# Blockwise attention and a swish feed-forward on one core: batch 0 in two passes by queries, K back on SyncE

## The reference

```python
scores = scale * np.matmul(q, k.transpose(0, 1, 3, 2))
mask = block_i >= block_j                    # blocks of 64 positions
attn = softmax(np.where(mask, scores, -1e9))
x = np.matmul(attn, v).transpose(0, 2, 1, 3).reshape(4608, 512)
h = x @ w_in                                 # 512 x 2048
g = h * (1.0 / (1.0 + np.exp(-beta * h)))
out = g @ w_out                              # 2048 x 512
```

## Time and profile before

| | |
|---|---|
| median of 3 runs | 364.31 us (364.09 to 367.67) |
| the profiled execution | 364.09 us |
| its span | 362.3 us |
| mean granted clock of TensorE | 0.967 |
| TensorE busy | 332.3 us |
| VectorE, ScalarE, GpSimd busy | 218.2, 211.0, 82.4 us |
| DMA | 53.41 MB |

### The profile page before, as it was taken

The page is one execution under the profiler, slowest core; times in us unless marked ns, Lnnn a source line. Parts: engine busy times, 40 slices in busy tenths (PEclk is TensorE's granted clock), DMA queues, the critical chain, the costliest instruction groups (busy, mean ns, idle before and its releaser), DMA issues.

```text
span 362.3 us, 7406 instructions
## 1 busy us (share of the span) xinstructions
PE 332.3 (92%) x3104; PEld 205.7 (57%) x3048; DVE 218.2 (60%) x447; ACT 211.0 (58%) x320; POOL 82.4 (23%) x127
## 2 busy tenths in 40 slices
PE   7879959876998999999956999999999999999996
PEld 5465345432556644765533566656666676676685
DVE  4657735354574548855952567467648757757742
ACT  2938906126955669668552876775687636535521
POOL 6684066303601804203703333000000000000000
PEclk9999969996999999999995999999999999999999
DMA  8999999999999599999799786150231021020023
GB/s 211 205 250 225 227 217 212 202 200 251 182 210 238 99 226 235 210 205 235 162 201 213 145 187 101 50 121 18 78 50 49 18 78 57 2 87 31 0 90 116
DMA packets 113313, 53.41 MB, mean 147 GB/s; under 512 B 83568, under 2 KB 112768, under 8 KB 113280
## 3 DMA queue, kind: packets, MB, share of 16 engines
q1 hardware_dynamic: 91424, 32.06, 46.3%
q10 hardware_dynamic: 16288, 16.52, 17.0%
q0 software_dynamic: 5568, 4.36, 7.6%
HBM read 36.71 MB, written 9.44 MB: 127 GB/s over the span
## 4 chain that ended last, share of the span: by engine, by line
PE 69%; DVE 6%; SPq 6%; DMA 6%; ACT 4%; POOL 3%; ACTq 3%; issue 2%; POOLq 0%
PE PS L960 28%; PE PS L890 24%; PE PS L747 7%; SPq L534 5%; PE PS L695 5%; PE PS L996 4%; DVE gT L974 3%; ACTq L1017 2%; DMA OV<-in_v_dram 2%; DMA xT<-xq 2%; ACT E L709 2%; DMA Vs<-in_v_dram 1%; DVE xq L766 1%; DVE OV L857 1%; ACT th L970 1%
## 5 line engine op out<-in xcount | busy, mean ns | idle before, releaser
L960 PE MATMUL PS<-xT,w_in 128*128 128x512 bf16 x576 | 143.3, 388 | 5.2 <-ACT ost L1011 4.7
L970 ACT ACTIVATE th<-PS,beta 128x512 f32<-128x512 f32 x144 | 97.2, 696 | 69.0 <-PE PS L960 66.1
L974 DVE SCALAR_TENSOR_TENSOR gT<-th,PS 128x512 f16<-128x512 f32 x144 | 95.9, 681 | 54.2 <-ACT th L970 53.9
L709 ACT ACTIVATE E<-PS 128x1024 bf16<-128x1024 f32 x93 | 92.1, 1031 | 42.4 <-PE PS L695 39.2
L960 PEld LDWEIGHTS PS<-xT,w_in 128*128 128x128 bf16 x576 | 53.6, 99 | 61.9 <-issue 6.0
L890 PE MATMUL PS<-w_out,gT 128*128 128x256 f16 x512 | 63.9, 273 | 0.0
L890 PEld LDWEIGHTS PS<-w_out,gT 128*128 128x128 f16 x512 | 48.6, 98 | 12.7 <-issue 0.8
L656 POOL CAST QKn<-ST 128x640 bf16<-128x640 f32 x48 | 35.5, 740 | 81.7 <-DMA ST<-in_k_dram 67.7
L747 PE MATMUL PS<-Vn,E 128*128 128x65 bf16 x930 | 35.2, 198 | 12.2 <-DMA xT<-xq 6.8
L747 PEld LDWEIGHTS PS<-Vn,E 128*128 128x128 bf16 x930 | 33.5, 101 | 17.8 <-DMA xT<-xq 7.1
L695 PE MATMUL PS<-QKT 64*128 64x512 bf16 (+4 forms) x328 | 37.6, 300 | 2.3 <-ACT E L709 2.0
(11 more groups left out here) (61 smaller groups left out, 176.3 us busy)
## 6 DMA issues: line engine op xcount, KB each, us to landing
out_dram<-ost ACTq DMA_DIRECT2D x36, 256.0 KB, 2.4
Vs<-in_v_dram SPq DMA_DIRECT2D x24, 256.0 KB, 6.1
ST<-in_q_dram SPq DMA_DIRECT2D x8, 288.0 KB, 6.3
ST<-in_k_dram SPq DMA_DIRECT2D x8, 288.0 KB, 6.8
w_in<-in_moe_w_in_dram POOLq DMA_DIRECT2D x4, 512.0 KB, 10.1
w_out<-in_moe_w_out_dram POOLq DMA_DIRECT2D x4, 512.0 KB, 10.3
OV<-in_v_dram SPq DMA_DIRECT2D x4, 256.0 KB, 12.3
Vs<-in_v_dram SPq DMA_DIRECT2D x6, 128.0 KB, 8.0
```

What stands on the lines that cost most here:

```text
L709: return g.activation(E3[es_(te)][:, g0, :, :], PS[:, ps.slot:ps.slot + 2, :], ACT.Exp, scale=0.125)
L960: z = g.matmul(PS[:, ph.slot, :], w_in[:, c, 128 * j:128 * j + 128], xT[:, c, row % RX:row % RX + RC], start=(c == 0), stop=(c == 3))
L970: return g.activation(th[tt.slot][:], PS[:, ph.slot, :], ACT.Tanh, scale=beta[:, j:j + 1])
L974: return g.scalar_tensor_tensor(out=gT[tg.slot][:, j, :], in0=th[tt.slot][:], scalar=1.0, in1=PS[:, ph.slot, :], op0=ALU.add, op1=ALU.mult)
```

## The change

- V of batch 0 comes on SP alone, in whole key tiles of all heads: part 0 is tiles 0 and 1, part 1 is the others. GpSimd casts each part for each pair.
- QK products of batch 0 are cut into nine blocks of 128 to 320 columns, laid out so that the first group holds all that queries 0 to 255 need. Its tiles of zeros move with them (CLEAR).
- PV, reciprocal, product, transpose and copy of batch 0 are done for query tiles 0 and 1 first (which wait for the first exponential and part 0 of V alone), then for tiles 2 to 4.
- Chunk 0's inner products are done for rows 0 to 255 (half 0, from the first passes), then for rows 256 to 511, two slices j in one PSUM bank, with two tanh of 256 columns each.
- K of batches 2 to 7 goes out on SP, behind Q. Q and K may use either of the two buffers.
- Pieces 1, 2 and 3 of w_in wait for K of pair 2, K of pair 3 and part 0 of V of batch 0; w_out waits for the last K of batch 1 and has a priority ahead of the casts of the last pairs.
- Both copies of xT that ScalarE did for batch 0 go to VectorE.

```diff
--- before.py
+++ after.py
-        PARTS = [((0, 4, "SP", range(6)), (4, 8, "SP", range(2)), (4, 8, "POOL", range(2, 6)))] + [((0, 8, "SP", range(6)),)] * 7
+        PARTS = [(range(0, 2), range(2, 6))] + [(range(6),)] * 7
...
+        BLOCKS = [{0: [(0, 0, 256, 0), (1, 128, 256, 256), (2, 384, 512, 384)], 1: [(0, 256, 576, 0), (3, 384, 576, 320)],
+                   2: [(1, 256, 576, 0), (2, 256, 384, 320), (2, 512, 576, 448)], 3: [(4, 512, 576, 0)]},
+                  {0: [(0, 0, 512, 0)], 1: [(0, 512, 576, 448), (1, 128, 576, 0)],
+                   2: [(2, 256, 576, 0), (3, 384, 576, 320)], 3: [(4, 512, 576, 0)]}]
+        CLEAR = [[(0, 256), (320,), (320,)], [(0,), (0,), (0, 320)]]
...
-            wout.append(P.op("POOL", 1000, fwo, xfer=3150, dma=(f"d_wout{a}", 1), prio=-18 if a < 1 else 4.6))
...
-            for h0, h1, e, tt in PARTS[b]:
+            for part, tt in enumerate(PARTS[b]):
...
-                    def fv(g, e, ts=ts, t=t, b=b, h0=h0, h1=h1, i=i):
-                        d = Vn[t.slot] if e == "POOL" else Vs[ts.slot]
...
-                            return [g.dma_start(d[:, i, h0:h1, 0:64],
-                                                v[b, h0:h1, 128 * i:128 * i + 128, :].rearrange("h p d -> p h d"))]
+                            return [g.dma_start(d[:, i, :, 0:64],
...
-                        o = P.op("SP", 300 + 550 * n, fv, tiles=[ts], xfer=(1400 if b == 0 else 1200) * n,
-                                 prio=3.5 + 0.1 * (h0 > 0) if b == 0 else 4 * b + (3.5 if b < 2 else 0.5),
-                                 dma=["d_V", h0, 1])
-                        o.pkt = 90.0
-                    else:
-                        o = P.op("POOL", 150 + 1450 * n, fv, tiles=[t], xfer=1400 * n, prio=-30 if b == 0 else 4 * b + (3.5 if b < 2 else 0.5), dma=["d_VP", h0, 1])
...
+                    o = P.op("SP", 300 + 550 * n, fv, tiles=[ts], xfer=(1400 if b == 0 else 1200) * n,
+                             prio=3.5 if b == 0 else 4 * b + (3.5 if b < 2 else 0.5), dma=["d_V", part, 1])
...
-                n = 5 if 4 in tt else len(tt)
-                for g0 in range(h0, h1, 2):
...
-                        return g.tensor_copy(Vn[t.slot][:, 0:n, g0:g1, 0:64], Vs[ts.slot][:, 0:n, g0:g1, :])
...
+                for g0 in range(0, 8, 2):
...
+                        return g.tensor_copy(Vn[t.slot][:, t0:t1, g0:g0 + 2, 0:64], Vs[ts.slot][:, t0:t1, g0:g0 + 2, :])
+
+                    o = P.op("POOL", 60 + 120 * (t1 - t0), fw, deps=[*vs, *ones, *vzero], tiles=[ts, t],
+                             prio=4 * b + 0.5 - (38.5 - 5 * part) * (b < 1))
...
                         ts = whole[w] = P.tile("S8")
-                        ts.only = (w,)
 
...
-                        o = P.op("ACT" if w else "SP", QKI, fl, deps=[o for t in early6 for o in t.users] if b == QB else [],
+                        o = P.op("SP", QKI, fl, deps=[o for t in early6 for o in t.users] if b == QB else [],
                                  tiles=[ts], xfer=QKX, prio=u, dma=["d_S8", 0, 1])
...
-                        if w:
-                            o.after = ld["Q", u]
...
-                        blocks = {0: [(0, 0, 512, 0)], 1: [(0, 512, 576, 448), (1, 128, 576, 0)],
-                                  2: [(2, 256, 576, 0), (3, 384, 576, 320)], 3: [(4, 512, 576, 0)]}[g0]
-                        for t, q0, q1, off in blocks:
+                        for t, q0, q1, off in BLOCKS[b > 0][g0]:
...
                 o = P.op("PE", n, fq, deps=cps, tiles=pst + [tqk] + [te] * (b > 0),
-                         lat=n + 200, mode="row", prio=pr(u) + .1 + .1*(grp[0] >= 2))
+                         lat=n + 200, mode="row", prio=pr(u) + (.1 + .1*(grp[0] >= 2) if b else -9 * (grp[0] == 0)))
...
-                    x = P.op("ACT", act_t(1024), fe, deps=[o], tiles=[ps, te], lat=act_t(1024) + 93, prio=0)
...
+                    x = P.op("ACT", act_t(1024), fe, deps=[o], tiles=[ps, te], lat=act_t(1024) + 93,
+                             prio=-1 if b == 0 and g0 == 0 else 0)
...
+                    cl = CLEAR[b > 0][g0]
+
+                    def fz(g, e, g0=g0, te=te, cl=cl):
+                        a = E3[es_(te)][64:128, g0, :, cl[0]:cl[0] + 64]
+                        if len(cl) == 1:
+                            return g.memset(a, 0.0)
+                        return g.memset(bass.AP(a.tensor, a.offset, [a.ap[0], [512, 2], [cl[1] - cl[0], 2], [1, 64]]), 0.0)
+                    zs.append(P.op("DVE", 110 + 55 * len(cl), fz, deps=[x], tiles=[te], prio=-20))
...
-            def eblk(te, t, i, h):
-                if t == 4:
+            def eblk(te, t, i, h, b=b):
+                if b == 0 and t < 4:
+                    g0, off = {(0, 0): (0, 0), (0, 1): (0, 128), (0, 2): (1, 0), (0, 3): (1, 128), (0, 4): (1, 256),
+                               (1, 1): (0, 256), (1, 2): (2, 0), (1, 3): (2, 128), (1, 4): (2, 256), (2, 2): (2, 320),
+                               (2, 3): (0, 384), (2, 4): (2, 448), (3, 3): (1, 320), (3, 4): (1, 448)}[t, i]
+                    a = 1024 * g0 + 512 * h + off
+                elif t == 4:
...
-            if u == 3:
+            if u == 7:
...
-            pv = P.tile("PP")
-            pv.at = (4, 6, 0, 2) if u == 3 else (4, 6) if b < 1 else (0, 2)
...
-                            z = g.matmul(o, eblk(te, t, i, h), Vn[Tv.slot][:, t, 2 * c + h, 0:65],
...
-            av = P.op("PE", 30 * 34, fav, deps=ex + zs + load[u], tiles=[te, Tv, pv, ti, tx],
-                      lat=30 * 34 + 180, mode="full", prio=pr(u)+.4 + 5 * (b < 1))
...
+            for i0, i1 in ((0, 2), (2, 5)) if b < 1 else ((0, 5),):
+                pv = P.tile("PP")
+                pv.at = ((4, 6) if i0 == 0 else (4, 6, 0, 2)) if b < 1 else (0, 2)
+                ti, tx = P.tile("inv"), P.tile("xq")
+                first = b < 1 and i0 == 0
...
+                        for i in range(i0, i1):
+                            for t in range(i + 1):
+                                o = PS[:, pv.slot + h, 65 * i:65 * i + 65]
+                                z = g.matmul(o, eblk(te, t, i, h), Vn[Tv.slot][:, t, 2 * c + h, 0:65],
+                                             start=(t == 0), stop=(t == i))
...
+                n = 2 * 34 * (sum(range(i1 + 1)) - sum(range(i0 + 1)))
+                av = P.op("PE", n, fav, deps=(ex[0:1] + zs[0:1] + load[u][0:1]) if first else ex + zs + load[u],
+                          tiles=[te, Tv, pv, ti, tx], lat=n + 180, mode="full",
+                          prio=pr(u) + .4 + (0 if b else 5 * (i0 > 0) - 8 * (i0 == 0)))
...
+                def both(pv, n0, n1, i0=i0, i1=i1):
+                    a = PS[:, pv.slot, 65 * i0 + n0:65 * i0 + n1]
+                    return bass.AP(a.tensor, a.offset, [a.ap[0], [512, 2], [65, i1 - i0], [1, n1 - n0]])
...
+                m = P.op("DVE", dve_t(128 * (i1 - i0)), fm, deps=[av, r], tiles=[pv, ti, tx], prio=0)
...
+                n = 66 * (i1 - i0)
+                xp = P.op("PE", n, fx, deps=nrm, tiles=[tx, px], lat=n + 170, mode="full",
+                          prio=pr(u) + .5 + (0 if b else 5 * (i0 > 0) - 8 * (i0 == 0)))
...
+                    for t0, n, x0 in [(0, 256, 0)] if i1 == 2 else [(256, 320, 256)] if i0 == 2 else pieces(b):
...
+                o = P.op("DVE", 520 if b else 350, fy, deps=[xp], tiles=[px], prio=0)
+                (xa if first else xt).append(o)
...
         win[0].deps += [ld["K", 0]]
-        for o in ld["VP", 0, 4]:
-            o.deps += [ld["K", 2]]
-        for w in win[1:]:
-            w.deps += ld["V", 0, 4] + (ld["VP", 0, 4] if w is not win[1] else [])
+        win[1].deps += [ld["K",2]]
+        win[2].deps += [ld["K",3]]
+        win[3].deps += ld["V",0,0]
         for w in wout:
-            w.deps += ld["V", 1, 0]
+            w.deps += [ld["K",7]]
...
-                for o in (ld["Q", u], ld["K", u])[:2 if b < QB else 1]:
+                for o in (ld["Q", u], ld["K", u]):
...
-                    seq += [o for h0, _, e, _ in PARTS[b] if e == "SP" for o in ld["V", b, h0]]
+                    seq += [o for part in range(len(PARTS[b])) for o in ld["V", b, part]]
...
-            for j in range(NJ):
+            for half in range(2) if r == 0 else ():
+                for j in range(1, NJ, 2):
...
+                    def fh(g, e, ph=ph, j=j, half=half):
+                        for i in range(2):
+                            for c in range(4):
+                                z = g.matmul(PS[:, ph.slot, HC * i:HC * i + HC],
+                                             w_in[:, c, 128 * (j + i - 1):128 * (j + i)],
+                                             xT[:, c, HC * half:HC * half + HC], start=(c == 0), stop=(c == 3))
+                        return z
+
+                    o = P.op("PE", 8 * mm(HC), fh, deps=(xd if half else xa) + [win[j // 4]], tiles=[ph, tg],
+                             lat=8 * mm(HC) + 170, mode="full", prio=1000 + 0.5 * j + 8 * half)
+                    hs.append(o)
...
```

(44 more changed lines are left out.)

96 lines of the change are left out of this document (58 added, 38 removed).

## The result

The changed kernel took 352.62 us (median of 4 runs, 352.17 to 353.98), the kernel before beside it 365.74 us (4 runs, 364.09 to 367.67): a ratio of 0.9646, 95% interval 0.9579 to 0.9713. The forecast was 352.0. The profiled execution took 352.18 us with a span of 349.7.

A forecast was written before the change was run, and what follows sets the result against it. TensorE's idle and slow-clock time, from three waits blamed on K loads on ScalarE's queue, was there to win; the DMA floor decided. Middle span 350.1 (345.3 to 354.9) plus 1.8 around it gave 352 us; range 343 to 367.

The forecast's parts named there:

- The three waits: TensorE's waits for V of batch 1, a ScalarE evacuation and xT, blamed on ScalarE's K loads: 24.6 us with slow clock.
- The third wait: TensorE's wait for batch 4's xT, until 193.2 us, blamed on K of batch 7 on ScalarE's queue: 6.8 us.
- One queue carries as much: K loads moved to SP's queue: about 220 GB/s by one queue or two, so no cost; bad-side bound 7.0 us.
- The DMA floor and its middle: DMA stream up to batch 4's xT: span 345.3 us if 9.6 us of gaps return, 354.9 if none; middle 350.1.
- The first pass at 20 us, inner products at 26 to 27, at no cost: Batch 0's PV and chunk 0: inner products 5 to 6 us sooner, extra work free, 0 to 4 us kept for range.
- Row halves: Chunk 0's inner products: 256-column matmuls cost nothing more; ScalarE's tanh 4 us more, a price only if first half late.
- Weights: w_out issued at about 36 us, V of batch 1 near 47; chunk 0's outer products fill the first wait's 4.6 us.
- (a): Rival: the first wait, near 45 us, stays as w_out takes K's place before V of batch 1; 359.5 us, chance 0.15.
- (b): Rival: queues share evenly, so only half of the 4.5 us at xT comes back; 354.2 us, chance 0.08.
- (c): Rival: DMA stream to batch 4's xT stays as long, so gains before 185 us are waited off; 363 us, chance 0.14.
- (d): Rival: slower, transposes wait 5.4 us behind K on SP, plus 2.8 us of clock, four times; 372 us, chance 0.19.
- The signs: Signs if right: store issues under 3 us, no low clock near 85 us, inner products before 28 us, w_out before 40.

The follow-up runs named there:

- (1): The kernel before with only K of batches 2 to 7 moved to SP: 348.87 us, 0.9657; again beside the changed kernel 350.33 us, 0.9689.
- (2): The changed kernel with K of batches 2 to 7 back on ScalarE's queue: 369.32 us, 1.0251 to the kernel before.
- (4): The kernel before with chunk 0's four stores issued by SP instead of ScalarE, K staying on ScalarE: 354.99 us, 0.9873.
- (7): The changed kernel with w_in pieces 1 and 2 waiting for part 0 of batch 0's V, piece 3 for part 1: 356.94 us, 0.9852.
- run 8: The changed kernel without batch 0's two passes and without row halves; V by key tiles, earlier weights, K on SP stay: 359.56 us, 0.9939.
- (5): The changed kernel with chunk 0's inner products over all 512 rows at once, two passes kept: 356.29 us, 0.9839.
- (6): The changed kernel with w_out waiting for V of batch 1 again, at its earlier priority: 353.77 us, 0.9764.
- run 3: The kernel before with each K load on ScalarE's queue issued as nine DMAs of 128 KB: 391.07 us, 1.0772.
- (9): The kernel before with K on SP and three xq buffers in place of two: 349.46 us, 0.9647.

## Why the prediction was right, step by step

**The three waits come from K on ScalarE's queue: shown for two.** With K on SP alone the wait for V of batch 1 and the wait for ScalarE go (1); with K back on ScalarE the long issue returns, and the change is slower than before (2). The middle wait needs only that ScalarE issues a store behind K (4). With the clock behind them the two cost 4.6 + 4.7 + 3.0 + 2.6 = 14.9 us, which by itself is enough for the gain. The third wait I read wrongly. It stands with K on SP, too: 5.0 and 10.1 us in two executions of K alone, 6.0 in the changed kernel, where it was 6.8.

**One queue carries as much: right.** 223 GB/s by SP alone at 172.5 to 177.5 us, 217 by ScalarE's alone. But 220 is not what the engines give at most: SP alone moved 274 GB/s at 32.5 to 35 us, and both queues 270 before. And the issue of K on SP, which I took at 0.72 us, stood 11.10 and 4.85 us in two places.

**The DMA floor and its middle: the number held by luck.** The 193.2 us of the sum is where the PV went on after its wait. I put that at 183.9 us and the rest at 166.2; measured are 181.31 and 168.4. One is 2.6 too long, the other 2.2 too short, and they cancel. What the DMA queues had moved up to that PV, before and after:

```profile
DMA packets 84667, 40.52 MB, mean 210 GB/s; under 512 B 62232, under 2 KB 84136, under 8 KB 84648
DMA packets 75797, 37.62 MB, mean 207 GB/s; under 512 B 54513, under 2 KB 75265, under 8 KB 75777
```

The rate is the same, so none of the gaps came back, where I counted on half of 9.6 us. The three low stretches did recover, but two opened, 73 GB/s for 7.5 us at 160 us and 53 for 6 us at 178 us, and against 220 these lose 5.0 + 4.6 = 9.6 us again. What the trace shows instead is that 2.90 MB less had moved when the PV went on, 13.8 us at 210 GB/s. I had only K of batch 7 in the sum, 4.5 us; the four loads of V issued at 175.53 us before are now behind the wait, too, at 182.71. The rest of the 2.90 MB I did not trace, and no run tests this order alone. The slow clock that I took out of the rest came back, 6.27 us of work x 0.43 = 2.7 us.

The floor of 345.3 us itself is not confirmed: one execution of K alone had a span of 344.1, too near to decide, and taking away the wait at 80 us made chunk 4 start sooner although the bytes stayed the same (4, on another chip). SP's transposes wait for TensorE's results, so as I read it a stall of TensorE is in the DMA stream, too.

**The first pass at 20 us, inner products at 26 to 27, at no cost: the term that was mis-sized.** "The bytes ahead of tiles 0 and 1 are nearly those ahead of heads 0 to 3 before, so the first pass starts at about 20 us too" failed by 2 us. It left out w_in, which the change itself puts ahead of V: with w_in behind V the first PV starts at 18.15 us (7). V's part 0 was cast from 21.68, TensorE had no other work and waited 3.78 us, and the half clock behind it cost 8.20 x 0.48 = 3.9 us. I kept 0 to 4 us for this part; these 7.7 us stand in the place that I called covered. Inner products came at 28.37, still 4 us sooner than before. Runs 8 and 1 give the balance: 9.2 us lost, 6.6 regained.

**Row halves: right.** At full clock eight products of 256 columns take 1.03 us, and so do four of 512; whole rows are no faster (5). ScalarE's 32 tanh take 517 ns each, 32 x 0.517 - 16 x 0.70 = 5.3 us more, where I took 4. TensorE's timeline, and the groups by line and shape:

```profile
31.98 1.03 PE L964 MATMUL PS<-xT,w_in 128*128 128x256 bf16 x8
...
198.96 1.03 PE L990 MATMUL PS<-xT,w_in 128*128 128x512 bf16 x4
```

```profile
L975 ACT ACTIVATE th<-PS,beta 128x256 f32<-128x256 f32 x32 | 13.4, 517 | 12.5 <-PE PS L964 12.5
...
L765 DVE TENSOR_TENSOR xq<-PS,inv 128x384 bf16<-128x384 f32 x4 | 2.2, 552 | 0.1
...
L765 DVE TENSOR_TENSOR xq<-PS,inv 128x256 bf16<-128x256 f32 x4 | 1.7, 422 | 0.1
```

Two pieces of a pair take 552 + 422 = 974 ns where one took 823: 0.6 us for four pairs, in the low part of the 0 to 3.3.

**Weights: the times nearly right, the cover wrong.** w_out was issued at 37.37 (36 forecast) and V of batch 1 was cast at 49.03 (near 47 forecast). TensorE is busy from 44 to 50 us, but not by chunk 0's outer products, which start at 57.73: inner products in halves and QK of batch 1 fill it. With w_out late no change of the time can be told (6).

**The rivals.** (a) fell: V's landing did not move, as it feared, but there is no wait near 45 us. (b) is 1.6 us from the measured time, so the time does not decide. The Trainium skill's rule named in the prediction, page "DMA: Bandwidth & Descriptors", section "Queues, rings and completion order", is one of packets, and by packets the traces agree with it in two places: 1237 to 1268 in run 3, and 398 to 395 at 45 to 47.5 us of the changed kernel, where w_out moved 0.39 MB and V 0.10 because its packets are a quarter as long. So I was wrong to ask it for an even share of bytes. A K issued whole took more than its share even so, 517 packets to 53. (c) is spoken against by 4, and by chunk 4 at 183.87 us for 195.74. (d) is there, but small: the transposes of xT stand behind K's issue at 166.73, and 6.0 us of waits with 2.7 us of clock remain, where it needed three waits of 8.2.

**The signs.** Store issues, the clock at 80 us, w_out and GpSimd's wait for K (25.8 us for 67.7) came as named; but its waits for V in Vs rose from 36.1 to 63.4 us, so that sign says little. Two did not: inner products after 28 us, by 0.4, and a stretch of 73 GB/s at 160 us.

What stays open: why TensorE still waits for xT with K on SP. Three buffers for xq remove a part of that wait and leave the time where it was (9). The waits that went cost 24.6 us with their clock, those that stand again 7.7 + 8.7 = 16.4, which leaves 8.2 of the 12.6 us won; the other 4.4 lie in shorter gaps that I did not allot (TensorE's idle time as a whole fell from 362.3 - 332.3 = 30.0 to 349.7 - 330.1 = 19.6 us). Nor was it tried which of V by tiles, the finer QK blocks and the earlier weights costs the 9.2 us of run 8.

## What to carry to other kernels

For each long wait ask which queue held the DMA engines then: here a large load on a second engine's queue added no throughput, kept the other queue's urgent load out and held up the next DMA that its own engine issued. Measure the parts of a compound change alone: here one edit gave it all, and the larger one gave nothing beside it. Compare like places before and after: a sum that comes out right can hold two errors that cancel. A forecast of a floor by one resource is weak where that resource may wait for the one that it is meant to bound.

## What the runs showed of the hardware

An issue of a DMA is not always short. One store behind 1.18 MB of K on ScalarE stood 7.23 and 7.78 us, three stores on SP behind a load of Q 7.51, and nine loads of 128 KB on ScalarE 12.00; with no K on its queue a store took 0.34 us. Transposes are long in any case: four on SP took 5.60 to 15.71 us before the change and 11.02 behind K after it. The Trainium skill, page "DMA: Bandwidth & Descriptors", section "Issuing engines are not separate DMA queues", says that issuing from several engines only saves the sequencer's time of issue. On throughput the trace agrees (274 GB/s by SP alone at 32.5 to 35 us after, 270 by SP and ScalarE before); the time of issue, though, was not saved: K's 0.72 us left SP and 7.23 us came to ScalarE.

Two queues took turns by packets in the two places named above, so the one with longer packets moved more bytes: w_out four times those of V. A whole K on ScalarE took ten packets for one of SP's; why is open.
